# Where one normalisation stage of a fused attention, Fourier and MLP kernel runs: low parts, a column swap and two row tiles are moved

## The reference

```python
X = np.fft.fft(x, axis=1)
X = np.fft.fft(X, axis=2)
mixed = np.real(X).astype(np.float32)
u = x + mixed
mu = np.mean(u, axis=-1, keepdims=True)
var = np.mean((u - mu) ** 2, axis=-1, keepdims=True)
un = (u - mu) / np.sqrt(var + 1e-06)
ch = np.maximum(un @ w_ch1, 0.0) @ w_ch2
return (u + ch).astype(np.float32)
```

## Time and profile before

| | before |
|---|---|
| device time, median of 3 runs | 688.76 us (687.22 to 689.47) |
| profiled execution: its own time | 687.45 us |
| profiled execution: span | 685.6 us |
| TensorE busy | 674.9 us, 98% of the span |
| VectorE, ScalarE, GpSimd busy | 50%, 40%, 34% |
| share of the chain that ended last | TensorE 95%, VectorE 4% |
| mean granted TensorE clock | 0.995 |

### The profile page before, as it was taken

One profiled execution on the slowest core, in us unless ns is written; L12 is line 12 of the kernel. 1 busy time (PEld: TensorE's weight loads), 2 busy tenths in 40 slices (PEclk: granted clock), 3 DMA queues, 4 the chain that ended last, 5 costly groups with the idle time before them and its releaser, 6 DMA issues.

```text
span 685.6 us, 9772 instructions
## 1 busy us (share of the span) xinstructions
PE 674.9 (98%) x3666; PEld 549.2 (80%) x3666; DVE 341.6 (50%) x662; ACT 276.2 (40%) x586; POOL 232.7 (34%) x253
## 2 busy tenths in 40 slices
PE   7899999999999999999999999999999999999998
PEld 6677776767676789888888888888888899988886
DVE  4887786877876649633113111141111489944300
ACT  5767676767767613111111111121111387734411
POOL 5745878658595050887200000000150070000000
PEclk8999999999999999999999999999999999999999
DMA  5563544425444101344000000010230620000111
GB/s 172 146 151 83 137 141 108 118 65 149 118 128 111 58 1 32 96 119 108 16 1 1 0 1 0 1 62 0 76 109 1 185 62 0 1 32 15 47 47 46
DMA packets 26494, 47.04 MB, mean 69 GB/s; under 512 B 3792, under 2 KB 10832, under 8 KB 26448
## 3 DMA queue, kind: packets, MB, share of 16 engines
q1 hardware_dynamic: 23392, 38.08, 19.9%
q0 software_dynamic: 2912, 7.95, 3.7%
q10 hardware_dynamic: 144, 0.39, 0.2%
HBM read 35.98 MB, written 3.15 MB: 57 GB/s over the span
## 4 chain that ended last, share of the span: by engine, by line
PE 95%; DVE 4%; ACT 0%; issue 0%; POOL 0%; DVEq 0%; POOLq 0%
PE ps L1616 19%; PE ps L1582 19%; PE ps L1664 10%; PE ps L1678 10%; PE ps L1375 10%; PE ps L1361 9%; PE ps L1345 6%; PE ps L1346 5%; PE ps L1462 2%; PE ps L1297 1%; PE ps L1390 1%; PE ps L1517 1%; PE ps L1432 1%; PE ps L1601 1%; PE ps L1314 1%
## 5 line engine op out<-in xcount | busy, mean ns | idle before, releaser
L1175 DVE SCALAR_TENSOR_TENSOR hid_l<-ps,hid_h 128x512 fp32r<-128x512 f32 x48 | 33.2, 691 | 196.6 <-ACT hid_h L819 196.6
L819 ACT ACTIVATE hid_h<-ps 128x512 fp32r<-128x512 f32 x48 | 28.7, 598 | 223.7 <-PE ps L1582 223.7
L1361 PE MATMUL ps<-cst,prob 128*128 128x128 f32 x576 | 81.3, 274 | 0.9 <-DVE pt L945 0.9
L1345 PE MATMUL ps<-k,q 80*128 80x384 f32 x192 | 75.5, 393 | 1.1 <-ACT prob L706 0.8
L1616 PE MATMUL ps<-w_h,hid_h 128*128 128x512 f32 x192 | 76.2, 397 | 0.0
L1616 PE MATMUL ps<-w_h,hid_l 128*128 128x512 f32 x192 | 75.5, 393 | 0.0
L1616 PE MATMUL ps<-w_l,hid_h 128*128 128x512 f32 x192 | 74.7, 389 | 0.0
L1361 PEld LDWEIGHTS ps<-cst,prob 128*128 128x128 f32 x576 | 67.4, 141 | 8.8 <-issue 1.8
L1375 PE MATMUL ps<-pt,v_n 128*64 128x384 f32 x384 | 68.8, 494 | 0.0
L1346 PE MATMUL ps<-k,q 128*128 128x384 f32 x192 | 66.1, 344 | 0.0
L937 DVE TENSOR_REDUCE row_min<-ps 128x1 f32<-128x768 f32 x64 | 61.0, 954 | 7.8 <-PE ps L1346 6.8
(11 more groups left out here) (181 smaller groups left out, 1451.0 us busy)
## 6 DMA issues: line engine op xcount, KB each, us to landing
w_raw<-in_moe_w_ch SPq DMA_DIRECT2D x24, 256.0 KB, 2.6
raw_d<-in_q SPq DMA_DIRECT2D x8, 384.0 KB, 3.4
v_n<-in_v SPq DMA_DIRECT2D x16, 192.0 KB, 2.5
out<-out_s SPq DMA_DIRECT2D x12, 256.0 KB, 2.0
raw_qk<-in_k SPq DMA_DIRECT2D x15, 192.0 KB, 3.2
raw_qk<-in_q SPq DMA_DIRECT2D x15, 192.0 KB, 3.6
q<-q SPq DMA_DIRECT2D x15, 192.0 KB, 3.2
k<-k SPq DMA_DIRECT2D x15, 192.0 KB, 3.7
```

Of the source, the lines that this page charges most:

```text
L1345: nc.tensor.matmul(bank, q2[s][0:D + C, cols], k2[s][0:D + C, keys], start=True, stop=False)
L1361: last = nc.tensor.transpose(ps[:, 4 + hf, j * P:(j + 1) * P], prob[t % 2][:, R * hf + j, :], ident)
```

## The change

VectorE makes batch 1's low parts earlier among the statistics of batch 0, the swap of batch 1 becomes a function `swap(b)` of its own and stands in front of the normalisation, and the first two of block 0's four normalised tiles are made by GpSimd.

```diff
+NORM_SPLIT = 2
@@ gpsimd
             fold_block(0, 3)
             fold_block(1, 3)
 
+            pool.wait_ge(norm_ready, 1)
+            pool.wait_ge(w1_low, W1_AHEAD + W1_EARLY)
+            for j in range(NORM_SPLIT):
+                nc.gpsimd.tensor_scalar(un[:, j, :], x[:, 0, j, :], ln[:, j, 6:7], ln[:, j, 10:11], ALU.subtract,
+                                        ALU.mult).then_inc(un_ready, 1)
+
             pool.wait_ge(mix_ready, B * UNITS)
@@ vector
+            def swap(b):
+
+                dve.wait_ge(mix_ready, UNITS * b + UNIT_ORDER[b].index(0) + 1)
+                for z in (z_h, z_l):
+                    nc.vector.tensor_copy(z[:, 0:KC + 1, 0], as_f32(z[:, 0:KC + 1, HALF])).then_inc(z_swapped, 1)
+
             def mix(b, n):
@@
-                if n == 0:
-                    for z in (z_h, z_l):
-                        nc.vector.tensor_copy(z[:, 0:KC + 1, 0], as_f32(z[:, 0:KC + 1, HALF])).then_inc(z_swapped, 1)
+                if n == 0 and b == 0:
+                    swap(0)
@@
-            def norm(blk):
+            def norm(blk, first=0):
                 if blk:
                     dve.wait_ge(un_turned, KT * blk)
-                for j in range(TBT):
+                else:
+                    dve.wait_ge(norm_ready, 1)
+                    dve.wait_ge(w1_low, W1_AHEAD + W1_EARLY)
+                for j in range(first, TBT):
@@
             z_low_part(1, 0)
+            z_low_part(1, 1)
             statistics(0, 0)
-            z_low_part(1, 1)
+            z_low_part(1, 2)
+            z_low_part(1, 3)
             statistics(0, 1)
-            z_low_part(1, 2)
+            z_low_part(1, 4)
             statistics(0, 3)
-            z_low_part(1, 3)
             statistics(0, 4)
             variance(0)
-            z_low_part(1, 4)
             deviation(0)
-            dve.wait_ge(norm_ready, 1)
-            dve.wait_ge(w1_low, W1_AHEAD + W1_EARLY)
-            norm(0)
+            swap(1)
+            norm(0, NORM_SPLIT)
             mix(1, 0)
             mix(1, 3)
             store_un(0)
```

## The result

The changed kernel took 692.88 us (median of 8 runs, 691.71 to 694.66), and the kernel before, run beside it on the same chip, 688.88 us (8 runs, 687.22 to 690.92). The ratio is 1.006, with a 95% interval of 1.0043 to 1.0077: slower by about 4 us. Forecast were 688.7 us (range 687.3 to 690.2) and no change that can be measured.

The account below looks back on a forecast made before the run. VectorE was taken to bound this short stage. TensorE gains 0.95 us at unit R, then loses 0.5 to 0.7 at `un_ready`, in one case 0.36 more: 0.12 faster to 0.06 slower, hence 688.7 us, range 687.3 to 690.2.

Parts of the forecast that it names:

- The nearest is its tensor-by-scalar operation on 128x512, 0.62: GpSimd's two normalisations, having no row of their own, were priced at 0.62 us each from this operation.
- the far bound of 1.65: Upper price of one GpSimd normalisation: its longest operation of this size, with two tensors read, 1.65 us.
- GpSimd's normalisation is dearer: Rival, chance 0.20: wait at the first transpose; at 1.30 an operation 1.4 us slower, 690.2 us, each further tenth 0.2.
- The sharing of the two engines: GpSimd's and VectorE's normalisations run one after the other; VectorE ends 0.28 us behind GpSimd's end.
- 269.64 or 269.90: Start of VectorE's mixes: 269.64 if VectorE goes first, 269.90 if GpSimd does; then `mix(1, 3)` delays TensorE by 0.36.
- the last low part: VectorE's last low part of batch 1 starts at 265.41, removing TensorE's first wait of 0.60 us and its restart.
- no idle time between the halves of unit 0 and 1: TensorE has no wait between batch 1's cosine and sine halves, near 266.6; 0.60 us was lost there.
- the reciprocal: VectorE's reciprocal, behind the statistics and ScalarE's root, starts at 268.08, 1.00 us later than before.
- VectorE idle: VectorE waits before the reciprocal for ScalarE's root, a round trip the old order hid behind the last low part.
- unit R: TensorE's work behind VectorE's casts starts at about 268.45, 0.95 us earlier than before.
- this gain is lost again at `un_ready`: TensorE loses about 0.5 to 0.7 us, restart included, waiting for the normalised tiles before the transposes.
- the forecast for this half, no change: Earlier low parts and casts, all normalisations on VectorE: MLP 0.1 us earlier to 0.3 later, ratio 1.000.

Follow-up runs that it names:

- first probe run: Eleven extra GpSimd operations of several forms on a dead 128x455 buffer, added to the kernel with only the new VectorE order; one execution, 689.4 us.
- the run with the filled wait: Changed kernel plus 20 unused TensorE matmuls of 384 columns in front of the transposes; 690.67 us, ratio 1.0034 to before.
- small operation first: Changed kernel plus one 8-element GpSimd operation of the same form ahead of its wait for the statistics; 693.72 us, ratio 1.0073 to before.
- order-only kernel: Changed kernel with its new order kept but all four normalisations on VectorE; 688.27 us, ratio 0.9995 to before.
- multiply-add: Changed kernel with GpSimd's two tiles made as x times reciprocal deviation plus a shift computed by VectorE; 688.25 us, ratio 1.0002 to before.
- constants: Changed kernel with 0.5 and 2.0 instead of the scalar columns in GpSimd's two normalisations; 692.31 us, ratio 1.005 to before.
- GpSimd alone: Kernel before, in its old order, with only the first two of four normalisations moved to GpSimd; 689.91 us, ratio 1.0016.
- one tile: Changed kernel with one normalised tile on GpSimd instead of two, three on VectorE; 688.88 us, ratio 1.0009 to before.

## Why the prediction was wrong

**The time was wrong because of one price.** The step that failed is "The nearest is its tensor-by-scalar operation on 128x512, 0.62: same operation, same size, one tensor read", with the far bound of 1.65 behind it. Name and size were the same, but the two arithmetic operations inside weren't, and GpSimd's time hangs on them: 0.59 for a pair of multiplications, 1.76 with a subtraction, on 455 elements. The forecast weighed columns and rounding, which matter little (0.15 for columns; on 128x455, multiply-multiply took 0.58 with a rounded output, in the fold at 252.76 of the first probe run, and 0.59 without), and never the operations. The bound was taken from the longest operation that the kernel happened to hold, which is no bound for a form that it doesn't hold. The Trainium skill, page "GPSIMD Engine Reference", section "4.1 Engine selection", calls GpSimd with one input roughly line-rate against VectorE: for pairs of multiplications (0.62, beside VectorE's 0.54) the trace agrees; for subtract-multiply, 1.76 on 455 elements and 2.06 on 512, it doesn't.

**A second term was missing: the fall of the clock.** The rival "GpSimd's normalisation is dearer" had the right place, wait and sign. Its own rule, 1.4 slower at 1.30 and 0.2 for each further tenth, gives 1.4 + 10.6 x 0.2 = 3.5 at the measured mean of 2.36; the run with the filled wait has 2.79. The other 2.35 of the 5.14 are TensorE's matmuls at 1.2 GHz behind the wait. No case of the prediction had this term; the longest wait that it worked out, behind operations of 1.30, was 1.9 (269.51 to 271.39). How much the fall costs varies with where it comes: 2.35 in that profiled execution, about 1.6 where the clock was low for 3.4 us (13.49 with the small operation first, against 11.92 with the wait filled).

**The sharing of the two engines** was forecast as strict turns, with VectorE blocked until 0.28 behind GpSimd. VectorE's two normalisations took 1.00, as long as alone, and GpSimd's first took 0.60 longer than its second. So VectorE seems to have had the first turn, and then it was not held up by a GpSimd operation under way until 272.44. The mixes began at 269.19 on the time scale of before, where the forecast had 269.64 or 269.90, so `mix(1, 3)` was never late; all of the loss came through `un_ready`.

**Right** were, each on the time scale of before (1.37 off the times above): the last low part at 265.41 (266.78); no idle time between the halves of unit 0 and 1; the reciprocal at 268.06 (269.43, forecast 268.08); VectorE idle for 0.28 before it; unit R at 268.42 (269.79, forecast 268.45), a gain of 0.98 against 0.95; and that this gain is lost again at `un_ready`. The order-only kernel shows that the forecast for this half, no change, was right.

**What is left open.** The profiled stage grew by 5.14, the medians differ by 4.0. The two profiled executions were not typical: that of before (687.45) lies 1.4 under its median, that of the changed kernel (694.37) 1.5 over its own; of their difference of 6.9, 1.37 lies before the stage, 5.14 in it and 0.4 behind it. Behind it there is one place: at 561.38 TensorE had waited for `xt_l` of VectorE, and its matmul started 1.08 behind the one before it, against 0.31 at the same place (554.11) in the kernel before. These 0.8 are partly won back behind it. They don't belong to the change: the profiled executions with multiply-add and with the order alone have the same 0.8 at that place, those with constants and with the small operation first have nothing. Where the clock falls, within the wait or behind it, and for how long, isn't fixed either (6.8 us in the changed kernel's profiled execution, 3.4 in those two), so the changed kernel's other executions may have lost less in the stage. They were not profiled, and their mean clocks can't tell. Why the clock fell within a wait of 3.55 after 1.9 us of it, and not in one of 2.06, stays open.

## What to carry to other kernels

Before pricing an instruction on an engine by a row of the same name, compare the arithmetic inside it as well as its size; if no row has the same operations, the range is open at the top, and one probe on an idle stretch of the engine settles it. When a change makes the bounding engine wait for one that was off the path, price the wait twice, once itself and once for what the clock may do behind it: here the second price was nothing up to a wait of 2.06 in the profiled executions, and 1.6 to 2.4 us from 2.92 on. If two tiles must leave VectorE, put them on the engine that is idle and cheap for that very form: ScalarE took 0.76 us each on average, GpSimd 1.05 as multiply-add and 2.36 as subtract-multiply.

## What the hardware showed

GpSimd's tensor-by-scalar time depends on the pair of operations, by a factor of three: on 128x455, 0.59 us for multiply-multiply, multiply-add and add-multiply; 1.76 to 1.80 for subtract-multiply and multiply-subtract; 1.78 and 2.04 for maximum-multiply; 1.36 to 1.38 for one addition or subtraction alone. An add-multiply with the negative mean should then be as cheap as the multiply-add; it wasn't tried in the stage.

TensorE's granted clock stayed at 1.00 behind waits of 0.92, 1.48 and 2.06 us, and stood at 0.50 for 3.4, 3.4 and 6.8 us within or behind waits of 2.92, 3.54 and 3.55. Each is one execution. No border can be read from this: by the mean clocks it probably fell in two of the ten executions with a wait of 1.48 too.

The lock between VectorE and GpSimd was weaker than a whole instruction. In the kernel with GpSimd alone, a cast of VectorE that meets GpSimd's operation is stretched from 0.16 to 0.54, far less than that operation lasts:

```profile
267.87 0.54 DVE L1125 CAST z_h<-z_h 128x3 fp32r<-128x3 f32 x1
```

With one tile, VectorE's three normalisations took 1.75 instead of 1.46, beside a GpSimd operation of 2.65. The Trainium skill, page "SBUF — State Buffer", section "SBUF: two separate sides", says that whichever starts first gets the shared ports for the whole instruction and the other fully blocks. That fits GpSimd's first operation, which started 0.13 behind VectorE's and took 0.60 longer, but not VectorE's delays of 0.29 and 0.38 beside GpSimd operations of over 2 us. Beside a cheap form it was blocked to the end: in the first set of probes a cast that meets the multiply-multiply of 254.61 to 255.20 ends 0.02 behind it.

```profile
254.69 0.53 DVE L1129 CAST z_h<-z_h 128x3 fp32r<-128x3 f32 x1 [1.63 <-PE ps L1487]
```

What part of a dear operation holds the ports stays open.
